# Windowed attention in blocks of 64 queries, two heads on the partitions, probabilities normalised on GpSimd

## The reference, cut to what matters

```
scores_l = scale * q @ k.T          where |pos_q - pos_k| < 16, else -1e9
scores_s = scale * q @ k_max.T + log(32)
a = exp(all - max);  a = a / (sum(a) + 1e-9)
out = a @ concat(v, v_mean)
x = heads side by side, (2, 768, 512)
h = relu(x @ w_in); conv over 3 tokens; h * sigmoid(conv) @ w_out
y = that;  out = y + relu(layernorm(y) * g @ w_ch1) @ w_ch2
```

## Time and profile before

| | us |
|---|---|
| median of 3 runs | 530.15 (530.12 to 531.16) |
| the profiled execution | 531.99 |
| its span, first to last instruction | 530.2 |
| TensorE busy | 509.2 (96%) |
| VectorE busy | 234.5 (44%) |
| ScalarE busy | 173.8 (33%) |
| GpSimd busy | 169.6 (32%) |
| granted clock of TensorE, mean | 0.994 of full |

### The profile page before, as it was taken

One profiled execution on the slowest core, in us unless ns is written; L12 is line 12 of the kernel. 1 busy time (PEld: TensorE's weight loads), 2 busy tenths in 40 slices (PEclk: granted clock), 3 DMA queues, 4 the chain that ended last, 5 costly groups with the idle time before them and its releaser, 6 DMA issues.

```text
span 530.2 us, 7083 instructions
## 1 busy us (share of the span) xinstructions
PE 509.2 (96%) x2545; PEld 417.3 (79%) x2545; DVE 234.5 (44%) x503; ACT 173.8 (33%) x417; POOL 169.6 (32%) x279
## 2 busy tenths in 40 slices
PE   4999699899899999999999999999999999999997
PEld 2677477578889999898788888888888888888885
DVE  6677585944986646755533131151121123111112
ACT  2588578677333335333511110120101121101010
POOL 5234647515999600004999950000000000000000
PEclk9999989999999999999999999999999999999999
DMA  7675757330212200000233300020000002000002
GB/s 170 145 164 138 169 123 193 86 106 1 80 40 81 79 1 1 1 0 1 80 120 119 115 5 1 1 80 0 1 0 0 1 0 80 0 2 0 1 0 79
DMA packets 58814, 30.02 MB, mean 57 GB/s; under 512 B 44416, under 2 KB 52892, under 8 KB 58396
## 3 DMA queue, kind: packets, MB, share of 16 engines
q1 hardware_dynamic: 58780, 29.58, 20.8%
HBM read 25.84 MB, written 3.15 MB: 55 GB/s over the span
## 4 chain that ended last, share of the span: by engine, by line
PE 85%; DMA 5%; DVE 3%; SPq 3%; POOL 2%; issue 1%; ACT 1%; DVEq 0%; POOLq 0%
PE bank L1020 8%; PE bank L1018 8%; PE bank L1019 8%; PE bank L1035 8%; PE bank L1037 8%; PE bank L1036 8%; PE bank L855 5%; DMA vblk<-in_v 5%; PE bank L909 4%; PE bank L907 4%; PE bank L908 4%; PE bank L966 4%; PE bank L967 4%; PE bank L968 4%; PE bank L892 2%; PE bank L841 2%
## 5 line engine op out<-in xcount | busy, mean ns | idle before, releaser
L658 DVE SCALAR_TENSOR_TENSOR h2l<-bank,h2h 128x512 fp32r<-128x512 f32 x48 | 33.2, 692 | 203.9 <-ACT h2h L816 203.9
L816 ACT ACTIVATE h2h<-bank 128x512 fp32r<-128x512 f32 x48 | 28.7, 598 | 220.6 <-PE bank L1020 220.6
L1035 PE MATMUL bank<-wch,h2h 128*128 128x512 f32 x192 | 75.5, 393 | 0.1
L1037 PE MATMUL bank<-wch,h2l 128*128 128x512 f32 x192 | 74.8, 389 | 0.0
L1036 PE MATMUL bank<-wcl,h2h 128*128 128x512 f32 x192 | 74.7, 389 | 0.0
L1018 PE MATMUL bank<-xnh,wch 128*128 128x512 f32 x192 | 74.7, 389 | 0.0
L1019 PE MATMUL bank<-xnl,wch 128*128 128x512 f32 x192 | 74.7, 389 | 0.0
L1020 PE MATMUL bank<-xnh,wcl 128*128 128x512 f32 x192 | 74.7, 389 | 0.0
L409 POOL TENSOR_TENSOR wcl<-wst,wch 128x256 fp32r<-128x256 f32 x64 | 52.2, 816 | 5.3
L407 POOL TENSOR_SCALAR wch<-wst 128x256 fp32r<-128x256 f32 x64 | 33.1, 517 | 65.0 <-PE bank L909 65.0
L855 PE MATMUL bank<-kTw,qT 128*128 128x368 f32 x96 | 44.4, 549 | 8.4 <-DVE mx L497 7.7
(11 more groups left out here) (94 smaller groups left out, 868.8 us busy)
## 6 DMA issues: line engine op xcount, KB each, us to landing
wst<-in_moe_w_ch SPq DMA_DIRECT2D x32, 256.0 KB, 2.9
qn<-in_q SPq DMA_DIRECT2D x16, 192.0 KB, 3.3
vblk<-in_v SPq DMA_DIRECT2D x4, 768.0 KB, 8.3
out<-y SPq DMA_DIRECT2D x11, 256.0 KB, 2.1
kn<-in_k SPq DMA_DIRECT2D x14, 192.0 KB, 5.6
vA<-in_v SPq DMA_DIRECT2D x16, 160.0 KB
wst<-in_moe_w_in SPq DMA_DIRECT2D x8, 256.0 KB, 3.1
wst<-in_moe_w_out SPq DMA_DIRECT2D x8, 256.0 KB, 2.8
```

What stands on the lines that cost most here:

```text
L1035: nc.tensor.matmul(o, h2h[:, m % 2, rows], vh, start=(j == 0), stop=False, skip_group_check=True)
L1037: ins = nc.tensor.matmul(o, h2l[:, m % 2, rows], vh, start=False, stop=(j == JF - 1), skip_group_check=True)
```

## The change

The attention is tiled anew. A block is 64 queries, with the first head's 64 queries and the second head's 64 queries on the 128 partitions of one score tile. For that the queries are stored block-diagonally (`qBD`: head h's channels on partitions 64h on, its queries in columns 64h on, zeros elsewhere), and one matmul of 120 columns (96 window keys, 24 summary keys, `kW`, now holding both heads' channels without zeros) gives the scores of both. Four blocks form a group, three groups a pair, and the loops run over n = 0 to 23.

The queries' copy is now two instructions of 64 partitions for each pair; the keys are copied from PSUM straight into the windows by VectorE (`window_keys`, three instructions), the summary keys by GpSimd (`block_keys`). The exponentials are multiplied by the reciprocal of their sum before the transpose, by GpSimd's `normalise` into `pn`, one instruction per block. `probs_t` is four transposes a group, `outputs` four matmuls with all 128 columns of values (`vW`) as stationary; of the 128 x 128 result the two diagonal quarters are used, by `x_high` and `x_low`, straight from PSUM. `broadcast`, the old `normalise` and `xf` are gone. The sums of the value blocks are made by a tree of five additions. `kn` and `qn` are doubled, the first loads of the queries are issued by ScalarE. In SP's order `load_vblk` comes behind the next pair's `load_k` and `load_q`; GpSimd makes one `split` behind each `normalise` from group 4 on. The order of TensorE's turn is `scores(n+2)`, `probs_t(n-1)`, `hidden` parts from group 20 on, `outputs(n-1)`, then the transposes of keys (second group of a pair) or queries (third).

```diff
+    QB = 64
+    NQ = S // QB
+    KEYS = QB + 2 * WIN
+    KW = KEYS + NB
+    GB = 4
+    GPP = NQ // GB
+    NG = NPAIR * GPP
...
             for p in range(2, NPAIR):
-                if p % 2 == 0:
-                    load_vblk(p // 2)
                 if p + 1 < NPAIR:
                     load_k(p + 1)
                     load_q(p + 1)
+                if p % 2 == 0:
+                    load_vblk(p // 2)
                 load_v(p)
                 load_vsum(p)
-                if p < 6:
-                    load_w(p - 2)
+                for n in {2: (0, 1), 4: (2,), 5: (3,)}.get(p, ()):
+                    load_w(n)
...
+            def normalise(n):
+                pool.wait_ge(r_done, n + 1)
+                if n >= 2:
+                    pool.wait_ge(pt_ready, n - 1)
+                for j in range(GB):
+                    nc.gpsimd.tensor_scalar(pn[:, n % 2, j], ex[:, n % 2, j], rinv[:, n % 2, j:j + 1], 1.0,
+                                            ALU.mult, ALU.mult).then_inc(n_done, 1)
...
+            block_keys(0)
+            for n in range(NG):
+                if n == 0:
+                    normalise(0)
+                    block_keys(1)
+                else:
+                    if n % GPP == 2 and n // GPP + 2 < NPAIR:
+                        block_keys(n // GPP + 2)
+                    normalise(n)
+                if n >= SPLIT_STEP:
+                    split(n - SPLIT_STEP)
...
+            def block_sums(it, adds):
+                for i in adds:
+                    if i == 0:
+                        dve.wait_ge(vblk_in, 16 * (it + 1))
+                    else:
+                        dve.wait_ge(vsum_raw, VADDS * it + i)
+                    m = BLK >> (i + 1)
+                    if i == VADDS - 1:
+                        if it >= 2:
+                            for c in range(2):
+                                dve.wait_ge(v_in[c], 16 * NVDMA * (it - 1))
+                        dst = vs[:, it % 2, None, :]
+                    else:
+                        dst = vblk[:, 0:m]
+                    nc.vector.tensor_tensor(dst, vblk[:, 0:m], vblk[:, m:2 * m], ALU.add).then_inc(vsum_raw, 1)
+                if adds[-1] == VADDS - 1:
+                    dve.wait_ge(vsum_raw, VADDS * (it + 1))
+                    nc.vector.tensor_scalar(vs[:, it % 2], vs[:, it % 2], 1.0 / BLK, None, ALU.mult).then_inc(vsum_done, 1)
...
+            for n in range(NG):
+                p, t = n // GPP, n % GPP
+                if n + 1 < NG:
+                    score_max(n + 1)
+                if n >= 3:
+                    x_low(n - 3)
+                if t == 2 and p + 2 < NPAIR:
+                    key_max(p + 2)
+                    window_keys(p + 2)
+                if n == 0:
+                    block_sums(0, range(VADDS))
+                if t == 0 and p % 2 == 1 and p + 1 < NPAIR:
+                    block_sums((p + 1) // 2, (0, 1))
+                if t == 1 and p % 2 == 1 and p + 1 < NPAIR:
+                    block_sums((p + 1) // 2, (2, 3, 4))
...
+                row_sums(n)
+                if n == 0:
+                    key_max(1)
+                    window_keys(1)
...
+            queries(0)
+            for n in range(NG):
+                p, t = n // GPP, n % GPP
+                exps(n)
+                if n == 1:
+                    queries(1)
+                if t == 0 and 1 <= p < NPAIR - 1:
+                    queries(p + 1)
+                if n >= 1:
+                    probs_out(n - 1)
+                if n >= 2:
+                    x_high(n - 2)
...
             def scores(n):
+                p = n // GPP
+                if n % GPP == 0:
+                    pe.wait_ge(kw_done, 3 * (p + 1))
+                    pe.wait_ge(ksb_done, p + 1)
+                    pe.wait_ge(q_done, p + 1)
+                    if p < 2:
+                        pe.wait_ge(zero_done, 7)
                 if n >= 2:
+                    pe.wait_ge(mx_done, GB * (n - 1))
+                for j in range(GB):
+                    b = block_of(n, j)
+                    ins = nc.tensor.matmul(ps_s[n % 2][:, KW * j:KW * (j + 1)], qBD[p % 2][:, b], kW[p % 2][:, b],
+                                           start=True, stop=True)
+                ins.then_inc(s_ready, 1)
             def probs_t(n):
                 if n >= 2:
                     pe.wait_ge(pts_done, n - 1)
+                for j in range(GB):
+                    pe.wait_ge(n_done, GB * n + j + 1)
+                    ins = nc.tensor.transpose(ps_pt[n % 2][0:KW, P * j:P * (j + 1)], pn[:, n % 2, j], ident[:])
+                ins.then_inc(pt_ready, 1)
+            def outputs(n):
+                p = n // GPP
+                if n % GPP == 0:
+                    pe.wait_ge(v_in[p % 2], 16 * NVDMA * (p // 2 + 1))
+                pe.wait_ge(pts_done, n + 1)
                 if n >= 2:
+                    pe.wait_ge(x_done, n - 1)
+                for j in range(GB):
+                    b = block_of(n, j)
+                    ins = nc.tensor.matmul(ps_o[n % 2][:, P * j:P * (j + 1)], vW[p % 2][0:KW, b],
+                                           pts[0:KW, n % 2, P * j:P * (j + 1)], start=True, stop=True)
+                ins.then_inc(o_ready, 1)
...
+            keys_t(1)
+            for n in range(NG):
+                p, t = n // GPP, n % GPP
+                if n == 1:
+                    probs_t(0)
+                if n + 2 < NG:
+                    scores(n + 2)
+                if n == 0:
+                    queries_t(1)
+                if n >= 2:
+                    probs_t(n - 1)
+                if n >= HID_STEP:
+                    if n == HID_STEP:
+                        pe.wait_ge(w_done, SPLIT_ATTN)
+                        pe.wait_ge(cols_done, 1)
+                        pe.wait_ge(x_done, GPP * PPB)
+                    hidden(0, [2 * (n - HID_STEP), 2 * (n - HID_STEP) + 1])
                 if n >= 1:
                     outputs(n - 1)
+                if t == 1 and p + 2 < NPAIR:
+                    keys_t(p + 2)
+                if t == 2 and p + 2 < NPAIR:
+                    queries_t(p + 2)
                 if n == COLS_STEP:
                     pe.wait_ge(consts_in, 32)
+                    pe.wait_ge(q_done, NPAIR)
+                    nc.tensor.transpose(ps_kq[:, 0:KD + 3 * KF], rows[:],
                                         ident[0:KD + 3 * KF, 0:KD + 3 * KF]).then_inc(cols_ready, 1)
+            probs_t(NG - 1)
+            hidden(1, range(KD))
+            outputs(NG - 1)
```

More of the change, by code:

```diff
@@ L316, in _ @@
             load_v(0)
-            load_q(1)
             load_vsum(0)
+            load_v(1)
+            load_vsum(1)
             load_k(2)
             load_q(2)
-            load_v(1)
-            load_vsum(1)
             sp.dma_start(rows[0:KD], g_ln.rearrange("(c p) -> c p", p=P)).then_inc(consts_in, 16)
@@ L385, in window_keys @@
[L385 to L401 removed]
+            link(nc.gpsimd.memset(band[:], 0.0))
@@ L554, in gate @@
                                         ALU.subtract).then_inc(hg_done, 1)
-            dve.wait_ge(pool_init, 1)
-            keys(0, 0)
-            keys(0, 1)
-            dve.wait_ge(kT_done, 2)
-            for piece in range(3):
-                if piece == 2:
-                    key_max(0)
-                    dve.wait_ge(ks_done, 1)
-                dst, src = window_piece(0, piece)
-                nc.vector.tensor_copy(dst, src).then_inc(kw0_done, 1)
-            block_sums(0, 0)
-            block_sums(0, 1)
+            dve.wait_ge(zero_done, 7)
@@ L568, in _ @@
+            nc.vector.memset(mask[:, 2, KEYS - WIN:KEYS], NEG / SCALE).then_inc(mask_done, 1)
+            key_max(0)
+            window_keys(0)
             dve.wait_ge(mask_done, 6)
             score_max(0)
-            for part in range(2, 4):
-                block_sums(0, part)
-            block_means(0)
-            score_max(1)
-            keys(1, 0)
-            keys(1, 1)
-            for n in range(NT):
-                p, t = n // T, n % T
-                if n + 2 < NT:
-                    score_max(n + 2)
-                if n % G3 == 1:
-                    row_sums(n // G3)
-                if n >= 9 and n % G3 == 0:
-                    x_low(n // G3 - 3)
-                if n >= 5 and n % G3 == 2:
-                    normalise(n // G3 - 1)
-                for pp, g in KEY_STEPS.get(n, ()):
-                    if g < 2:
-                        keys(pp, g)
-                    else:
-                        key_max(pp)
-                if n == NT - 2:
-                    dve.wait_ge(cols_done, 1)
-                    taps(0)
-                if 1 <= t < 5 and p % 2 == 1 and p + 1 < NPAIR:
-                    block_sums(p // 2 + 1, t - 1)
-                    if t == 4:
-                        block_means(p // 2 + 1)
-                if n == COLS_STEP:
@@ L719, in relu, with x_high @@
```

(15 more changed lines are left out.)

509 lines of the change are left out of this document (188 added, 321 removed).

## The result

The changed kernel took 537.18 us (median of 4 runs, 535.83 to 540.07) against 530.65 for the kernel before (530.12 to 532.43): ratio 1.0124, 95% interval 1.0074 to 1.0175, slower by 6.5. Forecast: slower, 539.4. Its profiled execution took 537.94 around a span of 535.9.

A forecast was written before the change was run, and what follows sets the result against it. TensorE was taken as the bound, with project(0)'s start deciding. Start 40, groups 73.5, transposes 7.4, hidden 2.3, weights 2.5, stalls 12, slow records 3 and remaining hidden 6.2 put it at 146.9, +9.2: 539.4 us, range 516 to 562.

The forecast's parts named there:

- The reading that only `project(0)`'s start counts: The part from project(0) on is unchanged, so each microsecond won or lost before attention's end reaches the end one for one.
- TensorE's work: Per group of four blocks in attention: 2.52 us in place of 3.68, at 0.12 a record, bounds 0.107 and 0.155.
- The wait for ScalarE: Outputs wait for ScalarE's copy of the transposed probabilities, 0.94 us a group: cycle 3.5, pair 12.0 against 12.3.
- the covered case: If other TensorE work covered the wait for ScalarE's copy, a group would take 2.6 us.
- The two stalls: VectorE waits 6.2 us for late vblk in steps 9 and 15; TensorE stalls 6 each, plus 1.5 each for slow records.
- Adds beside GpSimd: VectorE's tree of adds takes 2.4 us, or 5.0 when colliding with GpSimd over SBUF; hidden under the cycle either way.
- The weights: First weights are issued late; split(0) waits between normalise(4) and normalise(5), costing 2.5 us (0 to 4).
- The start: First three groups end at 40 us (38 to 42), against 33.5 for the first six tiles before.
- The sum: Terms add to project(0) starting at 146.9 us instead of 137.7, +9.2, giving 539.4 on the median.
- Rival A: Faster: vblk arrives in time, so both stalls and their slow records go, 524.4 us, or 518; chance 0.33.
- Rival B: TensorE's clock stays low because of a gap in each group: 579 us, or 550 to 565 if partly; chance 0.08.
- Rival C: No change: one stall of 6 us and a start at 38, within 1 us; chance 0.05.

The follow-up runs named there:

- e3: Changed kernel with block values of batches 2 and 3 issued before keys and queries, and scores placed between transposes and outputs: 520.65 us.
- e7: e3 with the four normalising instructions of a group moved from GpSimd to VectorE, behind its reciprocal: 526.25 us.
- e1: Changed kernel with SP issuing the block values of batches 2 and 3 ahead of keys and queries, at the start of iterations 3 and 5: 525.93 us.
- e5: e3 with VectorE's adds of the first block values directly behind the first window keys, ahead of the first score maxima: 515.53 us.
- e2: Changed kernel with TensorE's turn reordered: transposes of n-1, scores of n+2, then outputs of n-1: 535.79 us.
- e6: e3 with VectorE's reciprocals ahead of key maxima, window keys and adds, and GpSimd's normalising ahead of its block-key copy: 523.46 us.
- e10: e5 with VectorE's row_sums ahead of the block-value adds, only in turns that have adds: 516.22 us.
- e9: e5 with the first two weight loads issued by SP ahead of load_v(2): 513.41 us.
- e4: Kernel before the change, with block values of batches 2 and 3 issued ahead of keys and queries in iterations 3 and 5: 530.09 us.
- e11: e5 with the edits of both e9 and e10: 513.03 us.

## Why the prediction was right

*The reading that only `project(0)`'s start counts* held in every kernel: from there to the end of the span it is 392.4 to 392.6 in all thirteen traces.

*TensorE's work.* Score records start 0.112 apart (8 in 0.89), between the 0.107 and 0.12 that I had. A group is 2.5, as said.

*The wait for ScalarE* was 0.68 to 0.72, said 0.94; twice that in the group with the query copies, which I had called even. The pair came out at 11.51, said 12.0. The forecast that the shorter work is given back as waiting is right. But I had 2.6 a group for the covered case, and that is wrong: with the wait covered (e3) the pair takes 11.2 to 11.7. e7 shows VectorE close behind (a pair takes 12.5 to 13.1 there, with 4 x 3 normalising instructions more on it), and e3 GpSimd's blocks, which the transposes wait for one by one. I had VectorE's work at 9.2 to 10.5 a pair and compared that mean with the cycle, but the adds of two pairs fall into one, between steps that wait for each other.

*The two stalls* were the main term: said 6 each behind a wait of 6.2, measured 5.48 and 5.44 behind 6.8; the landing 8.3 said, 8.1 measured. e1 shows them to be cause and not company: 11.2 less. What follows them cost 2.5 and 2.3, said 1.5; the clock's part is 1.9 and 1.7, and the rest, GpSimd's pace at the first transposes, I had not named. Missed was the third wait, 1.62 at 42.10 with 2.3 behind it.

*Adds beside GpSimd.* Both bounds had them hidden, 2.4 to 5.0 for a tree. With GpSimd idle they took 2.72 for four (e5, at 9.49); beside its splits 2.43 and 1.16 for two each in e3 (85.70, 90.15), 3.6. The Trainium skill (GPSIMD Engine Reference, Key points) has VectorE and GpSimd collide where VectorE reads two inputs from SBUF. The sign agrees; the cost here is a third, and not the doubling of my upper bound. GpSimd paid as well: its split beside the first two took 1.57 (86.01) instead of 0.73.

*The weights.* Said 2.5 on the path; GpSimd waited 3.87 (50.09), but the pair with that wait takes 11.6 (48.23 to 59.86), 0.1 more than the steady one. Where TensorE comes there sooner the same wait cost it 1.68 (e1), 1.45 (e3) and 2.45 (e5). The term fits a kernel that has no other slack there.

*The start.* The first three groups ended at 39.6, said 40. The query transposes came at 24.11, said 21.7, the first outputs at 29.13, said 26.9; the next groups made it up. e5 shows the term that I named, the whole tree ahead of `row_sums(0)`, as the avoidable part.

*The sum* gave +9.2 and +5.8 was measured. By the balance above: start -0.4, pairs -5.2 (78.1 less 0.1 for the weights is 78.0; 73.5 + 7.4 + 2.3 = 83.2 was said), stalls -1.1, weights -2.4, what follows the stalls +1.8, third wait with what follows it +3.9: -3.4. So luck has a part in how near the time came. The terms that I had named add up to 5.8 - 3.9 = +1.9; the other 3.9 are a wait of the same kind that I had not. The direction stands without it, by 2 us and not by 9. What the prediction named as its refutation (groups each 2.6, no wait of VectorE for `vblk`, score records 0.155 apart) did not come.

*Rival A* had the right mechanism at the wrong odds: the values in time give 524.4, it said, and e1 measures 525.9. It failed on its condition, SP's issue, which came at 62.21 behind the loads of the next pair. *Rival B* did not come in the changed kernel's steady pairs (records 0.112 apart at gaps of 0.7), but the clock did stay low longer than the sum has it: for most of one pair in e1. That gaps between groups do it is not shown. e3, with the gaps closed, was low for less, and e2, with the same gaps closed, for more (0.63 in 66:80 against 0.76). *Rival C* is excluded by the interval.

Open: why the wait of 1.68 at 52.54 in e1 is followed by slow records up to the scores at 63.09, and the wait of 1.62 at 42.10 in the changed kernel by slow ones only from 44.08 to 48.23. No run here was made to tell.

## What to carry to other kernels

When an engine works in order, a late transfer is paid by everything queued behind its first user, and making the rest faster lengthens that wait: in e2 the stalls grew by 1.5 and 1.8. So take the stall away first (e1 alone was worth 11.2, e2 alone 1.4). Moving other work ahead of the wait is no cure either: in e6 and e10 the next thing in the queue was waited for instead. Ask of each load not only when its data is wanted but what SP must wait for before it can issue it: three moves of loads and adds that change no arithmetic, e1, e5 and e9, were worth 18 us in sum, and the change itself cost 6.5. The same move can be worth nothing elsewhere (e4), where the loads that it overtakes have no slack.

## What the hardware showed unexpectedly

- Behind waits of TensorE of 2.45 (44.61 in e5, granted clock 0.74 in 39:52) and 1.68 (52.54 in e1, 0.61 in 52:65) records ran at the low level, while 2.24 in the kernel before left them fast, and so did 2.35 at 35.96 in e11 (granted clock 1.00 in 26:39). The length of the last wait alone does not tell.
- Records at the low level can cost more than the wait ahead of them: in e1's pair of 16.5 instead of 11.5, with a granted clock of 0.61, 3.1 against 1.9.
- GpSimd scaled 120 columns by a per-partition value in 368 ns and VectorE in 278 ns, but the starts in a row are 343 and 193 ns apart (after, e7): 1.8 times.
- Four transposes behind a wait for GpSimd go at GpSimd's pace, 1.26 instead of 0.60 at full clock: a long record there is not a slow clock.
